# Attention cut into jobs of query tiles, with the first network's chunks at 256 and 320 tokens

## The chip, the cores and the metric
One core of a Trainium2 chip. The metric is the device time of one execution in microseconds; the kernel before takes 1015.93 us, the median of 3 runs (1014.83 to 1018.68).

## What is computed
Causal attention with a bias on 32 heads (batch 4 x 8 heads, 576 tokens, 64 wide), then two networks on the 2304 tokens of 512 values. All in float32.

```python
scores = scale * np.matmul(q, k.transpose(0, 1, 3, 2))
cum = np.cumsum(np.maximum(s, 0.0), axis=-1)
bias = -(cum[:, :, :, None] - cum[:, :, None, :])
scores = np.where(causal, -1000000000.0, scores + np.minimum(bias, 0.0))
attn = softmax(scores)          # exp(scores - max) / (sum + 1e-9)
x = np.matmul(attn, v)          # rearranged to (2304, 512)
h = np.maximum(np.maximum(x @ w1, x @ w2), x @ w3);  x = h @ w_out      # 512 -> 768 -> 512
y = ((x @ w_a) * (x @ w_b)) @ w_out2                                    # 512 -> 1536 -> 512
```

## The kernel before
Every float32 operand of a matmul is split into two parts that TensorE takes as float32r (hi and lo), so that a product is three matmuls (hi x hi, hi x lo, lo x hi) or, in attention, two with both parts stacked on the 128 rows of the contraction.

**Attention, a head at a time.** A head's 576 queries are 5 tiles of 128, 128, 128, 128 and 64 rows (`ROWS`), tile i against its `KEYS[i]` keys. VectorE splits q and k (`k_hi_copy` L720, `q_hi` L725, `split_k` L741, `split_q` L735). ScalarE writes the bias of each tile (`bias` L531, a Relu of the cumulative row, spread over 128 partitions by a DMA through `cum_dram`, with the tile's own value as bias), GpSimd puts the mask on the diagonal block (`mask` L470). TensorE makes the scores (L942, two matmuls a tile, four for the last), VectorE adds score and bias and reduces the extreme (`neg_scores` L755), ScalarE takes the exponential (L538), VectorE the reciprocal of the sums (L749), GpSimd multiplies (`normalise` L477), TensorE transposes 128x128 blocks, or 64-row ones in the last tile (L957), ScalarE and VectorE copy and split the transposes (`pt_hi` L548, L550; `pt_lo` L762, L766), TensorE multiplies with v (`output` L970), ScalarE and VectorE add the halves into `x_raw` (L558, L774). GpSimd also splits v (L489, L492).

**Slots.** All engines walk the same list of slots (`walk`). In slot n head n is scored and head n-1 is transposed and multiplied with v; head n+1's operands are prepared. Slots 0 to 8 hold attention alone. From slot 9 on four slots carry one chunk of 288 tokens of the first network: three with two of the 6 row blocks each (`up_part` L989, six parts of 12 matmuls a slot) and one with `down_part` (L1011, 72 matmuls). Attention's steps stand between the parts, and a part stands behind the last transposes, ahead of the output. Heads end at slot 32, so chunks 6 and 7 (slots 33 to 40) run alone. The order on each engine is written out by hand in its `slot` function; waits on semaphores are in the order of the instructions.

**Weights of the first network** come in 16 pieces of 768 columns: DMA into one of two buffers (`load_w1` L398), VectorE's copy `w1_hi` (L729), GpSimd's `w1_lo` (L483). Pieces 0 to 9 are split in slots 1 to 8, the rest in slots 9 to 11.

**Second network.** 6 chunks of 384 tokens (`CH2`), 12 row blocks each: 24 matmuls into `ab_ps` (L1073), then 12 into `out_ps` (L1084). The first network's result goes through DRAM (`y_dram`).

The output of a head, as it stands in the code:

```python
lo, hi = (0, SPLIT) if half == 0 else (SPLIT, SEQ)
todo = [(j, pt) for j in range(QT) if P * j < hi for pt in (pt_hi, pt_lo)]
for at, (j, pt) in enumerate(todo):
    q0 = max(lo, P * j)
    ins = nc.tensor.matmul(pv_ps[:, q0:hi], v_st[par][0:ROWS[j], j, :], ...)
```

## Time and profile before

| | |
|---|---|
| median of 3 runs | 1015.93 us |
| the profiled execution | 1014.57 us, span of its instructions 1012.6 us |
| TensorE busy | 972.7 us (96%), 6213 matmuls |
| VectorE, ScalarE, GpSimd busy | 481.4, 429.9, 237.1 us |
| granted clock of TensorE, mean | 0.976 of 2.4 GHz |
| moved by DMA | 64.11 MB |

Durations of instructions are those of one execution. A matmul's duration in the trace reaches over the start of the next, since they are pipelined; what one costs in a row of them is the distance of starts. "Busy" counts overlapping instructions once.

### The profile page before, as it was taken

What the parts mean: (1) busy time and instruction counts of PE and PEld (TensorE: products, weight loads), DVE (VectorE), ACT (ScalarE), POOL (GpSimd) and SP (SyncE); (2) the same over time, 40 slices, a digit from 0 to 9 for tenths busy, and PEclk for the clock granted to TensorE, in tenths of its full rate; (3) what the DMA queues carried; (4) which work ended last, traced back from release to release, by engine and by line L of the source; (5) the groups of instructions that cost most, each with busy time, mean ns of one, the idle gap of its engine ahead of it and who ended that gap; (6) DMA issues with size and microseconds to landing.
All of it is one profiled execution on the core that took longest, in us unless ns stands there. A gap on an engine that the chain in (4) does not pass through costs nothing.

```text
span 1012.6 us, 18390 instructions
## 1 busy us (share of the span) xinstructions
PE 972.7 (96%) x6213; PEld 942.9 (93%) x6213; DVE 481.4 (48%) x1151; ACT 429.9 (42%) x1070; POOL 237.1 (23%) x438
## 2 busy tenths in 40 slices
PE   3778799999999999999999999999999999999998
PEld 2666799999999999999999999999999999999998
DVE  6888788667667767664324543212112112112111
ACT  4677566666666666664133432112112112112111
POOL 4877864443443442441000000000000000000000
PEclk9976799999999999999999999999999999999999
DMA  7444542332332332300021431100100100100000
GB/s 190 115 128 131 139 123 67 90 78 74 80 83 69 82 96 52 102 8 24 1 102 60 153 125 47 62 0 0 62 0 8 54 0 16 46 0 26 5 0 31
DMA packets 31465, 64.11 MB, mean 63 GB/s; under 512 B 3712, under 2 KB 18048, under 8 KB 31424
## 3 DMA queue, kind: packets, MB, share of 16 engines
q1 hardware_dynamic: 31424, 63.60, 22.0%
q8 instruction: 21, 0.34, 0.1%
q14 instruction: 20, 0.16, 0.1%
HBM read 54.08 MB, written 9.51 MB: 63 GB/s over the span
## 4 chain that ended last, share of the span: by engine, by line
PE 88%; issue 0%; DVE 0%
PE bank L1073 30%; PE bank L989 23%; PE bank L1084 15%; PE bank L1011 8%; PE bank L970 5%; PE bank L942 5%; PE bank L957 4%; DVE soft L755 0%; DVE x_raw L774 0%; DVE o_stage L898 0%; DVE pt_lo L762 0%; DVE neg_max L755 0%
## 5 line engine op out<-in xcount | busy, mean ns | idle before, releaser
L888 DVE TENSOR_TENSOR g_raw<-bank,a_sb 128x384 f32<-128x384 f32 x72 | 40.2, 558 | 285.4 <-PE bank L1073 285.3
L989 PE MATMUL bank<-xs_hi,w_hi 128*128 128x288 f32 x576 | 174.1, 302 | 0.5 <-issue 0.5
L989 PE MATMUL bank<-xs_lo,w_hi 128*128 128x288 f32 x576 | 169.8, 295 | 0.0
L989 PE MATMUL bank<-xs_hi,w_lo 128*128 128x288 f32 x576 | 169.6, 294 | 0.0
L1073 PE MATMUL bank<-y_hi,w2b_lo 128*128 128x384 f32 x432 | 145.2, 336 | 0.0
L1073 PE MATMUL bank<-y_lo,w2b_hi 128*128 128x384 f32 x432 | 145.0, 336 | 0.0
L1073 PE MATMUL bank<-y_hi,w2b_hi 128*128 128x384 f32 x432 | 145.0, 336 | 0.0
L755 DVE CUSTOM_DVE_ANT_0 soft<-bank,soft 128x128 f32<-128x128 f32 (+4 forms) x160 | 86.4, 540 | 77.1 <-PE bank L942 53.5
L477 POOL TENSOR_SCALAR soft<-soft,rden 128x128 f32<-128x128 f32 (+4 forms) x160 | 99.0, 631 | 84.2 <-DVE rden L749 84.2
L538 ACT ACTIVATE soft<-soft,neg_max 128x128 f32<-128x128 f32 (+4 forms) x160 | 95.6, 598 | 43.6 <-DVE neg_max L755 43.4
L665 ACT ACTIVATE a_sb<-bank 128x384 f32<-128x384 f32 x72 | 35.3, 490 | 182.5 <-PE bank L1073 180.5
L989 PEld LDWEIGHTS bank<-xs_hi,w_hi 128*128 128x128 f32 x576 | 108.1, 188 | 3.5 <-issue 0.8
L989 PEld LDWEIGHTS bank<-xs_lo,w_hi 128*128 128x128 f32 x576 | 108.3, 188 | 0.8
L989 PEld LDWEIGHTS bank<-xs_hi,w_lo 128*128 128x128 f32 x576 | 108.2, 188 | 0.0
L669 ACT ACTIVATE g_hi<-g_raw 128x384 fp32r<-128x384 f32 x72 | 37.8, 525 | 163.8 <-DVE g_raw L888 163.8
L942 PE MATMUL bank<-k_hi,q_st 128*128 128x128 f32 (+2 forms) x192 | 75.7, 407 | 22.6 <-DVE neg_max L755 19.1
L531 ACT ACTIVATE soft<-cum_bc,cum_q 128x128 f32<-128x128 f32 (+4 forms) x160 | 90.0, 596 | 5.8 <-DMA cum_bc<-cum_dram 5.8
L548 ACT ACTIVATE pt_hi<-bank 128x256 fp32r<-128x256 f32 (+3 forms) x160 | 67.0, 420 | 56.1 <-PE bank L957 54.9
L470 POOL TENSOR_SCALAR_AFFINE_SELECT soft<-soft 128x128 f32<-128x128 f32 (+1 forms) x160 | 55.0, 355 | 138.9 <-ACT soft L531 130.8
L762 DVE TENSOR_TENSOR pt_lo<-bank,pt_hi 128x256 fp32r<-128x256 f32 (+3 forms) x160 | 73.0, 472 | 29.4 <-ACT pt_hi L548 24.2
L1073 PEld LDWEIGHTS bank<-y_hi,w2b_lo 128*128 128x128 f32 x432 | 81.2, 188 | 0.0
L1073 PEld LDWEIGHTS bank<-y_hi,w2b_hi 128*128 128x128 f32 x432 | 81.2, 188 | 0.0
(88 smaller groups left out, 2115.9 us busy)
## 6 DMA issues: line engine op xcount, KB each, us to landing
qk_raw<-in_qkT SPq DMA_DIRECT2D x64, 288.0 KB, 4.4
w_raw<-in_w SPq DMA_DIRECT2D x40, 384.0 KB, 3.4
cum_bc<-cum_dram SPq DMA_DIRECT2D x32, 288.0 KB, 3.4
v_raw<-in_v SPq DMA_DIRECT2D x32, 160.0 KB, 2.2
y_raw<-y_dram SPq DMA_DIRECT2D x6, 768.0 KB, 4.8
outT<-o_stage SPq DMA_DIRECT2D x24, 192.0 KB, 1.9
y_dram<-m_tmp SPq DMA_DIRECT2D x16, 144.0 KB, 1.8
y_dram<-h_raw SPq DMA_DIRECT2D x16, 144.0 KB, 1.8
```

Source lines behind the costliest of these rows:

```text
L470: nc.gpsimd.affine_select(out=diag, in_=diag, compare_op=ALU.is_ge, fill=masked, base=0, pattern=[[-1, r]], channel_multiplier=1).then_inc ...
L477: nc.gpsimd.tensor_scalar(part, part, rden[par][0:ROWS[i], i:i + 1], 1.0, ALU.mult, ALU.mult).then_inc(prob_done, 1)
L531: nc.scalar.activation(soft[par][0:ROWS[i], OFF[i]:OFF[i] + KEYS[i]], cum_bc[par][0:ROWS[i], 0:KEYS[i]], ACT.Relu, bias=cum_q[par][0:ROWS[ ...
L538: nc.scalar.activation(part, part, ACT.Exp, bias=neg_max[par][0:ROWS[i], i:i + 1], scale=-1.0, accum_out=sums[par][0:ROWS[i], i:i + 1]).th ...
L548: last = nc.scalar.activation(dst, src, ACT.Copy)
L755: nc.vector.tensor_tensor_reduce(part, score_ps[0:ROWS[i], at:at + KEYS[i]], part, 1.0, 3.0e38, ALU.add, ALU.min, neg_max[par][0:ROWS[i], ...
L762: last = nc.vector.tensor_tensor(pt_view(pt_lo, i, full), tr[:, 0:full * r].rearrange("p (j n) -> p j n", j=full), pt_view(pt_hi, i, full) ...
L942: ins = nc.tensor.matmul(score_ps[0:r, at + k0:at + k1], q_st[par][:, P * i:P * i + r], k[:, k0:k1], start=(part == 0), stop=(part == 1))
L989: ins = nc.tensor.matmul(up_ps[g], up1_w(w, f, g, kc), x[:, kc, :], start=(kc == 0 and at == 0), stop=(kc == KC - 1 and at == 2))
L1011: ins = nc.tensor.matmul(up_ps[j % 3], down1_w(w, f, j), h[:, f, :], start=(f == 0 and at == 0), stop=(f == FB1 - 1 and at == 2))
L1073: ins = nc.tensor.matmul(ab_ps[2 * (f % 2) + g], w2_cols(hi, f, (g * KC + kc) * P), y[:, kc, :], start=(kc == 0 and at == 0), stop=(kc == ...
L1084: ins = nc.tensor.matmul(out_ps[j], w2_cols(hi, f, 2 * KC * P + j * P), g[f % 2][:, :], start=(f == 0 and at == 0), stop=(f == FB2 - 1 and ...
```

## The change
- **Jobs.** Attention is 40 jobs instead of 32 heads: jobs 0 to 7 are heads 0 to 7 (batch 0) with query tiles 0 and 1 only (256 tokens), jobs 8 to 15 the same heads with tiles 2, 3 and 4, jobs 16 to 39 whole heads. Slots 0 to 8 are attention alone (`alone_slot`).
- **First network.** 8 chunks of 256 and 320 tokens in turn instead of 288. Chunk 0 starts at slot 9 and takes 8 slots, chunk 1 (slot 17) too: one row block a slot in six of them, half of the down part in two (`DENSE`). From slot 25 four slots a chunk, as before. Chunks 6 and 7 (slots 41 to 48) run alone.
- **Steps.** A slot has 6 steps; where it holds only three parts they stand at steps 0, 2 and 4, ahead of the transposes of that step. The output follows step 5. The weight pieces are split in slots 2, 4 (one each) and 8 to 14 (two each).
- **Bias as contraction rows.** `qk_st` has four planes: q_hi over q_lo, k_hi over k_hi; then the rows of the bias (cumulative sum and ones, hi and lo, 4 of the 64 upper rows, the others zero) over q_hi, and the same over k_lo. The scores hold the bias; `bias` and `mask` are gone, `neg_scores` adds a constant mask tile `causal` and scales by -SCALE. The four bias rows of all heads are made by VectorE at the start, go to DRAM and come back by two small DMAs a job (`load_bias`). GpSimd copies the upper halves (`upper`), ScalarE the lower (`lower`), VectorE subtracts twice (`split_q`, `split_k`).
- **Full shapes.** The last query tile is loaded as 128 queries from 448 on, of which the lower 64 partitions count (`TOP`, `QUERY`); its transposes and the last rows of v are 128x128 too.
- **Second network.** 5 chunks, four of 512 tokens and one of 256. Loops are unrolled, register waits are constants.

```diff
+N_JOBS = HEADS + N_HEADS
+EARLY_TILES, LATE_TILES = (0, 1), (2, 3, 4)
+    if n < HEADS:
+        return EARLY_TILES
+    return LATE_TILES if n < 2 * HEADS else tuple(range(QT))
-CH1 = SEQ // 2
+CHUNK = [((0, SPLIT), (SPLIT, SEQ))[c % 2] for c in range(N_CH1)]
+FIRST = [9, 17, 25, 29, 33, 37, 41, 45]
+DENSE = 2
-CH2 = 384
+CH2 = 512
+W1_PIECES = {2: [0], 4: [1], 8: [2, 3], 9: [4, 5], 10: [6, 7], 11: [8, 9], 12: [10, 11], 13: [12, 13], 14: [14, 15]}
...
             # scores
-                for k0, k1 in ((0, SPLIT), (SPLIT, SEQ)) if i == QT - 1 else ((0, KEYS[i]),):
-                    for part, k in enumerate((k_hi[par], k_lo[par])):
-                        ins = nc.tensor.matmul(score_ps[0:r, at + k0:at + k1], q_st[par][:, P * i:P * i + r], k[:, k0:k1],
+                    for part in range(2):
+                        ins = nc.tensor.matmul(score_ps[:, at + k0:at + k1], st[:, 2 * part, q0:q0 + P],
+                                               st[:, 2 * part + 1, k0:k1], start=(part == 0), stop=(part == 1))
...
             # transposes
-                    ins = nc.tensor.transpose(tr[0:w, j * r:(j + 1) * r], soft[par][0:r, at:at + w], ident[0:r, 0:r])
+                for j in reversed(range(i + 1)):
+                    ins = nc.tensor.transpose(tr[:, j * ROWS[i]:j * ROWS[i] + P], soft[m % 2][:, at:at + P], ident[:, :])
...
             # output: all 128 rows of v_st and pt
+                        ins = nc.tensor.matmul(pv_ps[:, q0:hi], v_st[m % 2][:, j, :],
+                                               pt[:, PT_STEP * j + q0:PT_STEP * j + hi],
...
             # reduction of the scores
+                nc.vector.tensor_tensor_reduce(scored(n, i), score_ps[TOP[i]:P, at:at + KEYS[i]],
+                                               causal[...], -SCALE, 3.0e38, ALU.add, ALU.min, ...)
...
             # start, VectorE
+            for b in range(2):
+                nc.vector.memset(qk_st[b][0:DH, 2:4, :].bitcast(F32), 0.0)
...
+            for b in range(2):
+                nc.vector.memset(qk_st[b][0:4, 2:4, :].bitcast(F32), 1.0).then_inc(st_init, 1)
...
             # TensorE, slots from 9 on
+                for step in range(STEPS):
+                    at = step if parts == STEPS else step // 2
+                    if parts == STEPS or step % 2 == 0:
+                        if rows:
+                            ups(n, at)
+                        else:
+                            down_part(c, downs[at])
+                    if live(m) and step in tr_step(m):
+                        transposes(m, tr_step(m).index(step))
+                    if live(n) and step in score_step(n):
+                        scores(n, 2 + score_step(n).index(step))
+                if live(m):
+                    output(m)
+                if live(n + 1):
+                    scores(n + 1, 0)
+                    scores(n + 1, 1)
```

## Rows read from the trace of the kernel before

**Rows 1.** Stages: length, busy us (instructions) of PE PEld DVE ACT POOL, clock, DMA
```profile
0.00:11.80 11.80, 1.91 (x9) 1.48 (x9) 6.61 (x20) 2.53 (x5) 1.42 (x10) 1.00 0.53 141
11.80:119.00 107.20, 80.81 (x343) 64.72 (x344) 87.07 (x216) 73.57 (x197) 82.76 (x131) 0.78 0.54 145
...
240.60:480.50 239.90, 239.90 (x1792) 232.00 (x1790) 158.59 (x434) 151.36 (x411) 89.96 (x189) 1.00 0.25 68
480.50:558.30 77.80, 77.25 (x579) 77.05 (x579) 25.97 (x52) 21.82 (x47) 0.00 (x0) 1.00 0.17 55
558.30:1012.60 454.30, 451.25 (x2592) 450.18 (x2591) 113.95 (x198) 100.77 (x195) 0.00 (x0) 1.00 0.11 35
```

**Rows 2.** The chain that ended last: its shares, then pieces (start, us, what)
```profile
PE 88%; issue 0%; DVE 0%
...
268.18 1.87 PE bank L970 x14
...
283.34 1.87 PE bank L970 x14
...
480.52 29.00 PE bank L989 x216
...
581.20 4.16 PE bank L1073 x24
...
1005.34 4.23 PE bank L1084 x24
```

**Rows 3.** TensorE in order of time in one mixed slot (start, us, instruction)
```profile
268.13 0.28 PE L970 MATMUL bank<-pt_lo,v_st 128*128 128x256 f32 x1
268.25 0.22 PE L970 MATMUL bank<-pt_hi,v_st 128*128 128x128 f32 x1
...
269.44 0.28 PE L970 MATMUL bank<-pt_lo,v_st 128*128 128x192 f32 x1
269.64 0.29 PE L970 MATMUL bank<-pt_hi,v_st 64*128 64x64 f32 x1
...
269.98 0.33 PE L942 MATMUL bank<-k_hi,q_st 128*128 128x128 f32 x1
...
278.39 0.60 PE L957 MATMUL bank<-ident,soft 128*128 128x128 f32 x4
278.75 0.36 PE L942 MATMUL bank<-k_hi,q_st 128*64 128x256 f32 x1
...
281.04 0.51 PE L957 MATMUL bank<-ident,soft 64*128 64x64 f32 x5
281.49 0.40 PE L989 MATMUL bank<-xs_hi,w_hi 128*128 128x288 f32 x1
```

**Rows 4.** Groups by line: instruction, count, busy us, mean ns, idle before and releasers
```profile
L531 ACT ACTIVATE soft<-cum_bc,cum_q 128x128 f32<-128x128 f32 (+4 forms) x160 | 90.0, 596 | 5.8 <-DMA cum_bc<-cum_dram 5.8
L755 DVE CUSTOM_DVE_ANT_0 soft<-bank,soft 128x128 f32<-128x128 f32 (+4 forms) x160 | 86.4, 540 | 77.1 <-PE bank L942 53.5 <-issue 15.6 <-POOL soft L470 6.1
L762 DVE TENSOR_TENSOR pt_lo<-bank,pt_hi 128x256 fp32r<-128x256 f32 (+3 forms) x160 | 73.0, 472 | 29.4 <-ACT pt_hi L548 24.2 <-ACT pt_hi L550 4.1
L741 DVE TENSOR_TENSOR k_lo<-qk_raw,k_hi 128x576 fp32r<-128x576 f32 x32 | 26.2, 820 | 0.0
L483 POOL TENSOR_TENSOR w_lo<-w_raw,w_hi 128x768 fp32r<-128x768 f32 (+1 forms) x16 | 30.6, 1911 | 0.0
```

**Rows 5.** VectorE at the start, in order of time
```profile
0.94 0.54 DVE L701 MEMSET x_raw<- 32x576 f32 x1 [0.94 <-PEq L1126]
...
11.76 0.29 DVE L755 CUSTOM_DVE_ANT_0 soft<-bank,soft 128x128 f32<-128x128 f32 x1 [1.75 <-POOL soft L470]
```

**Rows 6.** TensorE in a slot of attention alone: last transposes, then the output
```profile
98.44 0.49 PE L957 MATMUL bank<-ident,soft 64*128 64x64 f32 x5 [0.36 <-DVE pt_lo L762]
...
100.13 0.36 PE L970 MATMUL bank<-pt_hi,v_st 128*128 128x256 f32 x1 [0.55 <-issue]
```

**Rows 7.** DMA issues: line, engine, count, KB each, us to landing
```profile
w_raw<-in_w SPq DMA_DIRECT2D x40, 384.0 KB, 3.4
```

More of the change, by code:

```diff
@@ L590, in slot @@
                 if live(m - 1):
-                    other_half(m - 1, par == 0)
+                    other_half(m - 1)
+                if ahead_of(n) is not None:
+                    for kc in range(KC - 1):
+                        x_hi(ahead_of(n), kc)
+                if live(m):
+                    for k in range(len(tiles(m))):
+                        pt_hi_copy(m, k)
+                exp(n, 2)
+            def slot(n):
+                m = n - 1
+                c, e = place(n)
+                rows, downs, rest, ahead, early = rows_of(n), downs_of(n), rest_of(n), ahead_of(n), early_w2(n)
+                if live(m - 1):
+                    other_half(m - 1)
@@ L626, in slot @@
[L626 to L632 removed]
+                    if rows and i == 0 and rest is None:
+                        m_copy(c, rows[0])
+                    if len(rows) == 2 and i == 3:
+                        m_copy(c, rows[1])
@@ L840, in slot @@
+            def slot(n):
+                m = n - 1
+                c, e = place(n)
+                rows, downs, rest, ahead, early = rows_of(n), downs_of(n), rest_of(n), ahead_of(n), early_w2(n)
+                for piece in W1_PIECES.get(n, []):
+                    w1_hi_copy(piece)
+                neg_scores(n, 0)
+                if live(m - 1):
+                    x_add(m - 1)
                 if rest is not None:
                     x_lo(rest, KC - 1)
-                if before(up, down) is not None:
-                    h_lo_sub(*before(up, down))
+                if pending_row(n) is not None:
+                    h_lo_sub(*pending_row(n))
```

1052 lines of the change are left out of this document (509 added, 543 removed).

## The prediction, made before the changed kernel was run
> **What bounds the kernel now.** I read the table of stages first, then the chain of waits, then single slots of TensorE. The table [rows 1] cuts the 1012.6 us span into five parts: 11.8 us of start; 107.2 us in which attention runs with no matmul of the first network beside it (TensorE at a mean granted clock of 0.78, VectorE busy 87.07 us of it); slots that mix attention and the first network up to 480.5 us (four of its six chunks are in the third row: PE busy 239.90 of 239.9 us at clock 1.00); 77.8 us of chunks 6 and 7 of that network alone; 454.3 us of the second network. The chain [rows 2] is 88% TensorE. So from 119 us on TensorE is the bound and only fewer or cheaper matmuls help; before that it is a pipeline of five engines in which VectorE works 81% of the time, and there TensorE's time is partly thrown away. That is the place where time can be won: work of the first network put beside attention earlier.
>
> **TensorE's prices.** Chunk 6 does 216 matmuls of 288 columns in 29.00 us (134 ns each), the second network 24 of 384 columns in 4.16 us (173.3 ns) [rows 2]. The difference of 39 to 40 ns is 96 columns at 2.4 columns per ns, so one costs columns/2.4 plus a fixed 13.3 ns. That gives 120.0 ns for 256 columns, 146.7 for 320, 226.7 for 512. The 256-column matmul from 268.13 to 268.25 us agrees [rows 3].
> A full attention head in a mixed slot costs TensorE 283.34 - 268.18 = 15.16 us, less 72 x 0.1333 = 9.60: 5.56 us [rows 2].
>
> **Second network.** 6 chunks x 432 matmuls of 384 columns become 4 x 432 of 512 and 432 of 256. Before: 2592 x 0.1733 = 449.3 us. After: 1728 x 0.2267 + 432 x 0.120 = 391.7 + 51.8 = 443.5. **-5.8 us**, from 432 fewer fixed parts. What lies around (454.3 - 449.3 = 5.0 us, three of them the tail) stays. Bounds: if the fixed part grew with the columns (173.3/384 per column, 231.1 ns at 512) the gain would be 0, with none at 512 columns it would be 5.8 + 1728 x 0.0133 = 29; two widths on one line make me take -5.8. The wider evictions (up to four 512-column copies per chunk and engine) lie beside 8.2 us of matmuls per block: nothing.
>
> **First network alone.** Chunks of 256 and 320 columns keep the sum of columns and the number of matmuls: 288 x (0.120 + 0.1467) = 76.8 us against 77.8 with its waits. 0.
>
> **Full shapes.** The last query tile is 64 rows, and its matmuls use part of the array. The 64-row transposes: from 281.04 to 281.49 us, with 0.09 us lost in front (the last full matmul would end at 280.95) and 0.1 us behind; four full ones from 278.39 to 278.75, so five full ones are about 0.45 too; what goes is some 0.1 us [rows 3]. The two 64-row matmuls of the output: 269.44 + 0.10 to 269.98 is 0.44 us; two full-height ones, bounded by weight loads of about 0.11, take 0.22, and the first scores matmul behind them loses its 0.04. Together **-0.36 us** per full head, in 16 heads that lie in purely TensorE-bound slots (-5.8 us) and in the mixed slots below. 5.56 becomes 5.2. Bounds 0 to -0.6.
> The Trainium skill, "TensorE: Matmul & The Clock Gate", section "Back-to-back issue gap", speaks against this part: it lists up to 64 columns at about 60 cycles and 128 columns at 134, so five transposes widened from 64 to 128 columns would cost 5 x 31 ns = 0.15 us more by an estimate from that page, and 0.36 would shrink to 0.2. The rows show 0.09 us for a 64-wide and 0.09 for a 128-wide transpose [rows 3], so I go by the rows.
>
> **Bias as contraction rows.** It removes per head five Relu passes of ScalarE (90.0 us / 32 = 2.8 us), GpSimd's five masks and one copy, and the wait of mask and scores on them; VectorE's four passes of 576 columns (L741's takes 0.82 us) become two of the same width: at most -1.6 us, and as two of the four are plain copies and cheaper I take -1.1 [rows 4]. ScalarE and GpSimd each get a copy of up to 1152 columns (1.3 to 1.8 us). None of it is on TensorE's path in the old mixed slots, where all three had slack, so there it is worth 0; its worth is that slots may be shorter. Scores keep their number of matmuls.
>
> **Start.** VectorE gets four memsets of 1152 columns before the scan (one of 576 took 0.54 us [rows 5], so 1.0 each), four passes for the bias rows (2.4 us), then a larger store to DRAM and a reload. The old first score reduction starts at 11.76 us [rows 5] behind a similar bounce; mine at 15. **+3.3** (0 to +6, by how much of it hides behind loads).
>
> **Attention alone.** Before 107.2/9 = 11.9 us a slot. After: 8 slots with tiles 0 and 1 only, one (slot 8) with three tiles, two weight pieces and three splits of x. A two-tile slot: VectorE has at most 2/5 of L755 and L762 (0.9 + 0.7), two splits of 256 columns (0.9), x (0.4), reciprocal (0.35): 3.3 us, at 81% busy 4.1; two fifths of 11.9 is 4.8 [rows 1, 4]. The chain (transposes, two copies, output, scores, reduction, exp) doesn't shrink with the tile, so I take 4.6: 8 x 4.6 = 37, less 2 for the first; slot 8 costs 3/5 of 11.9 and 1: 8. The first network then starts at 15 + 35 + 8 = **58 us, where it was 119**.
>
> **The 16 new dense slots (9 to 24)**, chunks 0 and 1 at half density, 36 matmuls a slot.
> Slots 9 to 16: 36 x 0.120 = 4.3 us, three tiles 3.9 us (5.2 less two score tiles, two transposes and the first output half). The last transposes now stand directly ahead of the output with no matmuls between. In the old slots with nothing between but four scores, TensorE went from 98.44 (transposes) to 100.13 (output) [rows 6]: some 1.3 us idle if the scores are not there. 9.5 us. Six of these slots carry two weight pieces: GpSimd 2 x 1.9 us, and each buffer waits for 3.4 us of DMA before VectorE's copy, the first thing in its slot [rows 4, 7]. GpSimd sums to about 9.1 us. I take 10.3 there: 6 x 10.3 + 2 x 9.6 = 81.
> Slots 17 to 24: 36 x 0.1467 = 5.3, attention 5.2, the idle 1.3, waits of scores on reductions 0.2: 12.0 each, 96. VectorE needs some 8 us of 12.
> Chunk 2 thus starts at 58 + 81 + 96 = 235 us.
>
> **The rest of the mixed slots**: chunks 2 to 5, 16 slots: 72 matmuls each, 8 x 8.64 + 8 x 10.56 = 153.6, and 16 x 5.2 - 1.5 (the last has no scores) = 81.7. End at 470 us, where it was 480.5.
>
> **Sum** on the span: 470 + 77.8 + (454.3 - 5.8) = 996.5, against 1012.6: **-16**. The profiled execution took 1014.57 us (2 us around its span), so it would be 998.5; the median of the runs shown is 1015.93, some 1.4 above it, and I forecast **1000 us**. Most of the gain is not a gain in full: the 61 us earlier start are paid back by 177 us of dense slots that hold a quarter of the first network.
>
> **Rivals.**
> (a) *The dense slots run slowly because the clock falls.* They leave 1 to 2 us idle per slot, and in the old attention-only stage, where TensorE waits in every slot, the granted clock was 0.78 on the mean; with the two levels 2.4 and 1.2 GHz that is 1.2 GHz in 44% of the time [rows 1]. If half of the 8 to 10.5 us of TensorE work in each of the 16 slots ran at 1.2 GHz, each gets 4.7 us longer: +75, about 1075. It decides against the change at +16/16 = 1.0 us per slot, i.e. about one slot in five at the low clock throughout. Against it: here TensorE works 85% at full clock, there about half. The Trainium skill, "TensorE: Matmul & The Clock Gate" (section "HAM oscillation — how this bites in real kernels"), has waits between bursts of matmuls throwing the clock back; rows 1 agree for the stage before. Chance 0.13, most likely at 1018 to 1045.
> (b) *Muted:* shapes and widths bring nothing (+11.6), or weight pieces set slots 9 to 14 at 11.9: 1008 to 1016, say 1011. That full shapes don't remove the gaps, since the gap after each transpose group is of another kind, belongs here. Chance 0.17.
> (c) *Better:* two-tile slots at 4.1 (-4), no idle ahead of the output (-10 or so over 16 slots since the scores' waits overlap it), 985. For it: all helpers got lighter. Chance 0.18.
> (d) The forecast, 990 to 1008: 0.52.
>
> Range: 984 to 1022, which leaves out the rest of (a) and a little of (c). Half a percent (5 us) is about what can be told from no change. Faster takes (c), (d) and a third of (b): 0.76; same, the rest of (b), 0.11; slower 0.13.
>
> **What would show it.** Right: first matmul of the first network near 58 us; slots 17 to 24 near 12 us with one idle of 1.3 us ahead of the output's matmuls; granted clock 1.00 from there on; no 64-row matmul; 24 matmuls of 512 columns in 5.44 us; chunk 6 at 470. Wrong: clock under 0.9 between 60 and 235 us, waits of VectorE on the weight DMA in each slot from 9 to 14, a first reduction later than 18 us, or 512-column matmuls of 231 ns.

## The result, and the profile after

The changed kernel takes **1028.01 us** (median of 4 runs, 1027.53 to 1028.70) beside 1016.44 us for the kernel before on the same chip: ratio **1.0113 [1.0092, 1.0134]**. It is 1.1% slower, where the forecast was 1000 us in a range of 984 to 1022.

TensorE has less to do than before and the kernel is longer all the same: 5776 matmuls instead of 6213, busy 949.7 us instead of 972.7. The page of the kernel after, its first section and its chain:

```profile
PE 949.7 (93%) x5776; PEld 864.0 (84%) x5776; DVE 475.4 (46%) x1059; ACT 393.9 (38%) x896; POOL 221.6 (22%) x306
PE 87%; issue 5%; DVE 3%; DMA 1%; ACT 1%; POOL 1%; SPq 0%; ACTq 0%; POOLq 0%; DVEq 0%
```

Before, from 113 us on (its 88% of the span), the chain was almost TensorE's alone [rows 2]. The chain after is followed to the start, and 11% of the span on it are other engines and "issue". To see where, the stages of the kernel after (columns as in [rows 1]: length, busy us and count of PE, PEld, DVE, ACT, POOL, granted clock, DMA):

```profile
16.50:66.80 50.30, 27.31 (x96) 21.25 (x97) 36.57 (x107) 25.10 (x73) 29.04 (x46) 1.00 0.46 142
66.80:160.50 93.70, 75.53 (x533) 71.94 (x532) 68.31 (x147) 49.59 (x112) 62.26 (x62) 0.95 0.34 106
160.50:266.30 105.80, 89.83 (x619) 83.69 (x617) 72.06 (x183) 63.62 (x157) 43.83 (x66) 1.00 0.21 66
266.30:501.20 234.90, 234.86 (x1795) 233.04 (x1794) 153.82 (x392) 135.29 (x340) 79.86 (x121) 1.00 0.18 54
...
579.00:1026.30 447.30, 443.81 (x2161) 376.19 (x2159) 107.80 (x164) 95.11 (x165) 0.00 (x0) 1.00 0.11 36
```

These are: attention alone, slots 9 to 16, slots 17 to 24, the four-slot chunks and the second network; the first network alone, left out here, is 77.8 us. From the fourth row on TensorE is hardly ever idle (3.5 us in the second network). In the second and third row it idles 18 and 16 us.

The same work in the kernel before has to be cut elsewhere. When its slot 17 starts, heads 0 to 15 and chunks 0 and 1 are done; after, that is the state at 266.3 us:

```profile
0.00:240.30 240.30, 204.02 (x1254) 183.36 (x1255) 182.64 (x466) 155.75 (x417) 146.87 (x249) 0.90 0.43 115
240.30:480.50 240.20, 240.20 (x1794) 232.30 (x1792) 158.82 (x436) 151.54 (x412) 90.26 (x190) 1.00 0.25 68
```

| like for like | before | after | |
|---|---|---|---|
| heads 0 to 15, chunks 0 and 1 | 240.3 | 266.3 | **+26.0** |
| heads 16 to 31, chunks 2 to 5 | 240.2 | 234.9 | -5.3 |
| first network alone | 77.8 | 77.8 | 0 |
| second network | 454.3 | 447.3 | -7.0 |
| span | 1012.6 | 1026.3 | +13.7 |

Behind 266.3 us the change won about what was forecast. The first quarter lost 26 us, though TensorE was busy for less time in it (193.87 us of the first 266.30 after, 204.02 of the first 240.30 before) and its granted clock was higher (0.98 beside 0.90).

### The profile page after: what moved, and what is told of

Its sections match the earlier page's. It is cut to its first block, busy times and chain, and to the rows that moved or that the text cites. A ratio compares the mean times of both kernels' runs of the same rounds, so it can differ in the third digit from the quotient of the medians.

```text
span 1026.3 us, 15198 instructions
## 1 busy us (share of the span) xinstructions
PE 949.7 (93%) x5776; PEld 864.0 (84%) x5776; DVE 475.4 (46%) x1059; ACT 393.9 (38%) x896; POOL 221.6 (22%) x306
## 4 chain that ended last, share of the span: by engine, by line
PE 87%; issue 5%; DVE 3%; DMA 1%; ACT 1%; POOL 1%; SPq 0%; ACTq 0%; POOLq 0%; DVEq 0%
PE bank L1047 29%; PE bank L946 21%; PE bank L1062 14%; PE bank L965 7%; PE bank L898 6%; PE bank L928 6%; PE bank L914 4%; DVE soft L723 1%; DMA w_raw<-in_w 1%; DVE qk_st L690 1%; ACT qk_st L495 1%; POOL w_lo L460 0%; POOL soft L454 0%; DVE qk_st L696 0%; DVE pt_lo L732 0%
## 5 line engine op out<-in xcount | busy, mean ns | idle before, releaser
L946 PE MATMUL bank<-xs_hi,w_hi 128*128 128x256 f32 (+1 forms) x576 | 174.3, 303 | 0.7 <-ACT h_raw L543 0.7
L946 PE MATMUL bank<-xs_hi,w_lo 128*128 128x256 f32 (+1 forms) x576 | 171.3, 297 | 0.0
L946 PE MATMUL bank<-xs_lo,w_hi 128*128 128x256 f32 (+1 forms) x576 | 171.3, 297 | 0.0
L454 POOL TENSOR_SCALAR soft<-soft,rden 128x576 f32<-128x576 f32 (+4 forms) x160 | 93.0, 599 | 257.2 <-DVE rden L709 257.2
L898 PE MATMUL bank<-qk_st 128*128 128x256 f32 (+4 forms) x384 | 97.8, 367 | 45.6 <-DVE neg_max L723 16.5
L1047 PE MATMUL bank<-y_lo,w2b_hi 128*128 128x512 f32 (+1 forms) x360 | 132.5, 368 | 0.0
L1047 PE MATMUL bank<-y_hi,w2b_hi 128*128 128x512 f32 (+1 forms) x360 | 132.5, 368 | 0.0
L1047 PE MATMUL bank<-y_hi,w2b_lo 128*128 128x512 f32 (+1 forms) x360 | 132.5, 368 | 0.0
L504 ACT ACTIVATE soft<-soft,neg_max 64x576 f32<-64x576 f32 (+4 forms) x160 | 96.1, 601 | 78.3 <-DVE neg_max L723 77.2
L723 DVE CUSTOM_DVE_ANT_0 soft<-bank,causal 64x576 f32<-64x576 f32 (+4 forms) x160 | 86.5, 540 | 59.9 <-PE bank L898 58.5
L928 PE MATMUL bank<-pt_hi,v_st 128*128 128x320 f32 (+4 forms) x224 | 61.3, 297 | 26.9 <-issue 24.8
```

The source lines that it names most:

```text
L454: nc.gpsimd.tensor_scalar(part, part, rden[n % 2][:, i:i + 1], 1.0, ALU.mult, ALU.mult).then_inc(prob_done, 1)
L504: nc.scalar.activation(scored(n, i), scored(n, i), ACT.Exp, bias=neg_max[n % 2][TOP[i]:P, i:i + 1], scale=-1.0, accum_out=sums[n % 2][TOP[ ...
L723: nc.vector.tensor_tensor_reduce(scored(n, i), score_ps[TOP[i]:P, at:at + KEYS[i]], causal[TOP[i]:P, ZERO + P - KEYS[i]:] if i < QT - 1 el ...
L898: ins = nc.tensor.matmul(score_ps[:, at + k0:at + k1], st[:, 2 * part, q0:q0 + P], st[:, 2 * part + 1, k0:k1], start=(part == 0), stop=(pa ...
L928: ins = nc.tensor.matmul(pv_ps[:, q0:hi], v_st[m % 2][:, j, :], pt[:, PT_STEP * j + q0:PT_STEP * j + hi], start=(at == 0), stop=(at == len ...
L946: ins = nc.tensor.matmul(up_ps[g][:, 0:width1(c)], up1_w(w, f, g, kc), x[:, kc, 0:width1(c)], start=(kc == 0 and at == 0), stop=(kc == KC ...
```

## Where the first quarter went: two readings

**A loop that goes once around in each dense slot.** The chain of waits through one of slots 17 to 24 in the kernel after, from one output (L928) to the next:

```profile
197.99 1.94 PE bank L928 x14
...
200.47 1.76 PE bank L946 x12
...
203.81 0.19 ACT soft L504
...
205.46 0.75 DVE qk_st L690
206.24 0.42 DVE pt_lo L732
...
207.32 0.80 PE bank L898 x4
208.12 1.76 PE bank L946 x12
209.88 0.55 PE bank L914 x5
210.43 1.10 issue
211.52 1.94 PE bank L928 x14
...
214.05 1.15 ACT qk_st L495
215.22 0.48 ACT h_hi L538
```

211.52 less 197.99 is 13.53 us, the length of slots 18 to 22 (the first and the last two of the eight are shorter, the mean is 13.1 to 13.2). Two of the slot's three groups of 12 first-network matmuls lie on this chain, one on that of the next slot; between them it passes through VectorE, ScalarE and "issue". In the next slot it leaves TensorE right behind the output and four scores, for ScalarE's L495. What releases ScalarE stands in its own rows, again in order of time, with the idle time and its releaser in brackets:

```profile
199.97 0.65 ACT L518 ACTIVATE pv_tmp<-bank 64x576 f32<-64x576 f32 x1 [1.72 <-PE bank L928]
200.64 1.17 ACT L495 ACTIVATE qk_st<-qk_raw 64x1152 fp32r<-64x1152 f32 x1
```

The head of ScalarE's queue in a slot is `other_half`, the copy of the output just made. It waits for the last matmul of the output, and the copy of the next job's operands (`lower`, L495), the split of the first network's row block and the exponentials stand behind it. VectorE's h_lo and second reduction wait for that, then the exponentials, the transposes' copies, the last scores, the last transposes and the output again. TensorE is busy 11.29 us of such a slot, the loop lasts 13.5. With 72 first-network matmuls a slot (chunks 2 to 5) TensorE's own work is longer than the loop, and it doesn't show.

**GpSimd's subtraction holds VectorE.** Two equal passes of VectorE on 64x256, then what GpSimd did, in a slot with one weight piece:

```profile
36.19 0.42 DVE L690 TENSOR_TENSOR qk_st<-qk_raw,qk_st 64x256 fp32r<-64x256 f32 x1
36.53 2.02 DVE L696 TENSOR_TENSOR qk_st<-qk_raw,qk_st 64x256 fp32r<-64x256 f32 x1
```
```profile
36.23 2.04 POOL L460 TENSOR_TENSOR w_lo<-w_raw,w_hi 128x768 fp32r<-128x768 f32 x1 [0.68 <-DVE w_hi L701]
```

The second pass lasts until 0.28 us after the end of GpSimd's. In slots 9 to 14 there are two pieces. Slot 10 is the longest of them (13.3 us, the others 11.6). Its subtraction of the next job's q (L690) stands ahead of the third reduction (L723) and is held; in slot 11, with the same list, L690 starts 0.45 us earlier in its slot, between GpSimd's two passes, and gets through in 0.57 us, and the k pass (L696) is held, behind that reduction. VectorE's rows of slot 10, then of slot 11:

```profile
84.18 1.81 DVE L690 TENSOR_TENSOR qk_st<-qk_raw,qk_st 64x320 fp32r<-64x320 f32 x1
86.02 0.76 DVE L723 CUSTOM_DVE_ANT_0 soft<-bank,causal 64x576 f32<-64x576 f32 x1
...
97.06 0.57 DVE L690 TENSOR_TENSOR qk_st<-qk_raw,qk_st 64x320 fp32r<-64x320 f32 x1
...
98.36 1.60 DVE L696 TENSOR_TENSOR qk_st<-qk_raw,qk_st 64x576 fp32r<-64x576 f32 x1
```

GpSimd's pass for slot 10 runs from 82.01 to 85.64, and the held one ends 0.35 us after it. The delayed reduction delays its exponential, behind which ScalarE's `pt_hi` copies are queued, and so the output: TensorE idles 3.24 us ahead of it in slot 10 and 1.57 in slot 11.

```profile
82.01 3.63 POOL L460 TENSOR_TENSOR w_lo<-w_raw,w_hi 128x768 fp32r<-128x768 f32 x2
```
```profile
89.86 0.38 PE L928 MATMUL bank<-pt_hi,v_st 128*128 128x320 f32 x1 [3.24 <-issue]
```

L690 is late where TensorE's clock falls early in the slot. Stages of one slot each (from one reciprocal of VectorE to the next): slots 10, 11 and 12 of the kernel after, then slot 11 of the run with 384 columns below, whose code is the same up to the second network:

```profile
76.53:89.87 13.34, 10.10 (x67) 9.69 (x67) 9.13 (x19) 5.98 (x13) 8.73 (x8) 0.87 0.49 148
89.87:101.52 11.65, 10.08 (x67) 9.68 (x67) 8.89 (x19) 5.86 (x13) 9.10 (x8) 0.85 0.34 101
101.52:113.10 11.58, 8.80 (x67) 8.26 (x67) 9.23 (x20) 5.99 (x13) 9.02 (x8) 1.00 0.42 129
88.92:102.48 13.56, 10.35 (x67) 9.81 (x67) 9.28 (x20) 5.75 (x13) 8.94 (x8) 0.87 0.48 148
```

In slots 9 to 14 of the kernel after the granted clock falls to 1.2 GHz for a stretch three times, at 77.1, 90.7 and 114.6 us, each time soon after TensorE had been idle for 1.9 to 3.2 us ahead of an output. Where the stretch begins within 0.6 us of the slot's start the scores come late, L690 meets GpSimd's second pass, and the slot takes 13.3 to 13.6 us; where it begins later (slots 11 and 13) the slot stays at 11.6. At clock 1.00 none of slots 9 to 14 was longer than 11.7 in either run. In the profile with 384 columns four slots, 11 to 14, are long, and the six together last 77.1 us instead of 71.3, with the same code: a single profile is no sure measure of these slots.

These gave the first theories. T1: the weight pieces' subtraction on GpSimd makes the early slots long. T2: slots 17 to 24 are a loop through the output. The rival to both was that VectorE or ScalarE simply have too much in these slots, and for the second network that its gain comes from something other than the width.

## The experiments

All are edits of the kernel after, except where the kernel before is named. Times are medians, ratios are to the kernel before on the same chip; the kernel after is at 1028.01 and 1.0113. The kernel before had medians of 1014.51 to 1016.65 us on the chips of these runs, so differences of medians between kernels of different chips are sure to about 2 us only, and the ratios are to be preferred. Line numbers shift by a few with an edit. "Slots 17 to 24" is read from the distance of VectorE's reciprocals (0.19 us each, one a slot).

### 384 columns in the second network
```diff
-CH2 = 512
+CH2 = 384
```


> The changed kernel with the second network's chunks set back to 384 tokens (six chunks instead of five), all else as changed. By the sum of the prediction the 432 matmuls more cost 13.3 ns each: +5.8 us against the changed kernel, about 1034 us. Rival: the wider evictions or the larger loads had taken the gain away, then 0 (about 1028).

1035.92 us, 1.0194 [1.0164, 1.0223]. TensorE's blocks of 24 matmuls are 4.16 us in this kernel and 5.44 in the kernel after (chain of waits).

The second network takes 452.3 us (585.86 to 1038.2) instead of 447.3: the width is worth **5.0 us**. The other 2.0 of the 7.0 come with the rest of the change to that part (unrolled loops, constant waits); they were not tested apart. The rest of the 7.9 us between the medians lies ahead of 579 us, which this edit doesn't touch. In the profiled execution (1040.28 us, the longest of the four) that part is 6.9 us longer: slots 11 to 14 take 13.4 to 13.6 us at clock 0.87, as told above.

### Low parts of the weights by VectorE, right behind its copy
```diff
             def w1_hi_copy(piece):
...
+                dve.wait_ge(w1_hi_done, piece + 1)
+                nc.vector.tensor_tensor(w1_lo[:, cols], w1_raw[piece % 2][:, :], w1_hi[:, cols].bitcast(F32),
+                                        ALU.subtract).then_inc(w1_lo_done, 1)
...
-                for piece in W1_PIECES.get(n, []):
-                    w1_lo_sub(piece)
```


> The changed kernel with the low parts of the first network's weights subtracted by VectorE right behind its copy, instead of by GpSimd. Theory 1: GpSimd's 1.9 us subtraction holds VectorE's subtractions up (2.03 us instead of 0.42 for a split in the slots with a piece), and that sets the slots with pieces: slots 2 and 4 get 1.5 us shorter each, slot 8 by 2, slots 9 to 14 by about 1 each, in all -9 to -13 us (about 1017), although VectorE gets 16 x 0.95 = 15 us more work. Rival: VectorE's own load or the weight DMA sets these slots, then 0 to +8 us.

1038.67 us, 1.0228 [1.0196, 1.0259]: worse. Slots 2 and 4 with one piece are 0.5 us or so shorter, but slots 9 to 14 take 12.5 to 15.5 us instead of 11.6 (12.5 and 13.0 in slots 9 and 10, at clock 1.00; 13.6 to 15.5 in the four others, at 0.78 to 0.88). Slots 17 to 24 are untouched at 13.55. So the place matters: two copies and two subtractions at the head of VectorE's queue stand in the loop. This doesn't refute the hold; it shows that the repair can't stand there.

### ScalarE's `lower` behind the first copy of the transposes
```diff
-                if live(n + 1):
-                    lower(n + 1)
...
                         pt_hi_copy(m, tr_step(m).index(i))
+                    if live(n + 1) and i == 0:
+                        lower(n + 1)
```
(VectorE's two splits stand one step later.)

> The changed kernel with ScalarE's copy of the lower halves (1.15 us) moved from the head of its slot to behind the first copy of transposes, and VectorE's two splits one step later each; only in slots from 9 on. Theory 2: in slots 17 to 24 the chain copy, h_hi, h_lo, second reduction, exp, m_copy, pt_hi, pt_lo, split, fourth reduction, last scores leaves TensorE idle 2 us a slot in the middle; with the copy and a split out of it these 8 slots fall from 13.5 to 11.6 to 12.2 us: -10 to -15 us in all (about 1015). Rival: other work in the same queues takes their place, under -4 us.

1026.81 us, 1.0100 [1.0069, 1.0131]; slots 17 to 24 alternate between 12.5 and 13.6 us. It takes 1.15 us off the queue's head and brings about one.

### A part of the matmuls behind the last transposes
```diff
-                    at = step if parts == STEPS else step // 2
-                    if parts == STEPS or step % 2 == 0:
+                    at = step if parts == STEPS else {0: 0, 2: 1, 5: 2}.get(step)
+                    if at is not None:
```


> The changed kernel with the third part of 12 matmuls in slots 9 to 24 moved from ahead of the last transposes to behind them. Theory 3: nothing covers the two copies between the last transposes and the output (TensorE idle 1.1 to 3.2 us there in each slot); with 1.4 or 1.8 us of matmuls in between, 16 slots get 1.1 to 1.4 us shorter, -18 us (about 1010). Rival: these slots are set by VectorE's and ScalarE's order, so TensorE's wait only moves to the scores or transposes: under -5 us.

1024.71 us, 1.0095 [1.0062, 1.0128]; slots 18 to 22 are 13.03 us instead of 13.53. The gap of 1.1 us ahead of the output is filled, and half a microsecond comes of it.

### Both


> The changed kernel with both edits of the two runs before: the copy and splits later, and the third part of matmuls behind the last transposes. Alone they brought 1 and 3 us. Theory 2+3 (each wait stands in the other's shadow): slots 17 to 24 have 5.3 us of chunk, 5.2 of attention and some 1 us left, 11.6 to 12 each instead of 13.5, and slots 9 to 16 lose 0.5 each: -14 to -18 us, about 1012. Rival: the effects add and no more, -4 to -5 us, then what sets these slots is neither.

1028.12 us, 1.0122 [1.0096, 1.0148]; slots 18 to 22 are 13.3 us. Together they bring nothing. ScalarE's head of the queue still stands waiting for the output, now for 3.38 us where it was 1.72. In this profile the clock also fell to 0.89 in slot 25, which took 15.8 us instead of 14.2; that is more than the 1.1 us that slots 17 to 24 won together.

```profile
201.53 0.65 ACT L518 ACTIVATE pv_tmp<-bank 64x576 f32<-64x576 f32 x1 [3.38 <-PE bank L928]
```

### No low parts at all
GpSimd writes zeros in place of the low parts of the first network's weights, so that part of the computation is left out.
```diff
-                nc.gpsimd.tensor_tensor(w1_lo[:, cols], w1_raw[piece % 2][:, :], w1_hi[:, cols].bitcast(F32),
-                                        ALU.subtract).then_inc(w1_lo_done, 1)
+                nc.gpsimd.memset(w1_lo[:, cols].bitcast(F32), 0.0).then_inc(w1_lo_done, 1)
```


> The changed kernel where GpSimd writes zeros for the low parts of the first network's weights instead of subtracting (this leaves out the low parts of these weights): one write-only pass in place of one that reads two operands from SBUF. Theory 1: the subtraction holds VectorE's passes up. The splits in slots 2 and 4 fall from 2.03 us to 0.42 to 1, slots 2, 4 and 8 get 1.5 us shorter each, and slots 9 to 14 by 0.5 to 1.5: -8 to -13 us. Rival, that VectorE's order alone or the DMA of the pieces sets them: under -3 us.

1020.87 us, 1.0054 [1.0035, 1.0073]: 7.1 us less. Slots 2 and 4 take 6.1 and 4.85 us (7.7 and 6.6 after), slot 8 takes 9.7 (12.1). Slot 10 falls from 13.3 to 11.6, and no slot from 8 to 14 has a clock under 1.00. But the others of slots 9 to 14 stay at 11.6 (slot 9 at 11.2). Their chain has no weight piece in it; it is the loop of slots 17 to 24 with fewer parts:

```profile
83.81 1.15 ACT qk_st L494
...
87.11 0.80 PE bank L897 x4
...
91.76 1.77 issue
```

T1 holds for slots 2, 4, 8 and 10 and fails, on this evidence, for the rest of slots 9 to 14.

### Full height of the output in the kernel before
```diff
+            for pt in (pt_hi, pt_lo):
+                nc.vector.memset(pt[DH:P, (PT_STEP + P) * (QT - 1):].bitcast(F32), 0.0)
...
-                    ins = nc.tensor.matmul(pv_ps[:, q0:hi], v_st[par][0:ROWS[j], j, :],
-                                           pt[0:ROWS[j], PT_STEP * j + q0:PT_STEP * j + hi],
+                    ins = nc.tensor.matmul(pv_ps[:, q0:hi], v_st[par][:, j, :],
+                                           pt[:, PT_STEP * j + q0:PT_STEP * j + hi],
```


> The kernel before with one part of the change alone: the last two matmuls of each head's output at the full height of 128 rows, over zeros, instead of 64. By the sum of the prediction 0.22 to 0.26 us less in each of the 23 heads that lie in slots bound by TensorE, and less than that in the 9 alone: -5 to -6 us, ratio 0.994 to 0.995. Rival: the lost time belongs to the wait of the weight loads and stays: 0.

1006.29 us (1005.26 to 1008.34), 0.9909 [0.9884, 0.9935]: **8.2 us from one matmul call of the kernel before**, and two memsets at the start that put zeros into the rows it now reads. The same stretch as in [rows 3], TensorE in order of time:

```profile
267.44 0.27 PE L972 MATMUL bank<-pt_lo,v_st 128*128 128x192 f32 x1
267.56 0.22 PE L972 MATMUL bank<-pt_hi,v_st 128*128 128x64 f32 x1
...
267.72 0.30 PE L944 MATMUL bank<-k_hi,q_st 128*128 128x128 f32 x1
```

From the 192-column matmul to the scores 0.28 us, where it was 0.54 [rows 3]: 0.26 us a head. In 24 heads beside the first network that is 6.2 us, and chunk 6 starts 6.2 us earlier (474.34 us, before 480.52 [rows 2]). Next to nothing lies behind that: the two profiled executions differ by the same 6.2 us (1008.34 and 1014.57), and the other 2.0 are the scatter of the runs, the profiled one of 1008.34 being the longest of its four.

### Full density from slot 13 and 21 on, attention alone between
```diff
-FIRST = [9, 17, 25, 29, 33, 37, 41, 45]
-DENSE = 2
+FIRST = [13, 21, 25, 29, 33, 37, 41, 45]
+DENSE = 0
...
-    return list(range(STEPS // 2 * (e - FB1), STEPS // 2 * (e - FB1 + 1))) if c < DENSE else list(range(STEPS))
+    return list(range(STEPS)) if e == 3 else []
```


> The changed kernel with the jobs as they are but chunks 0 and 1 at full density: chunk 0 in slots 13 to 16 and chunk 1 in slots 21 to 24, two row blocks a slot, and slots 9 to 12 and 17 to 20 attention alone. Theory 4: a slot has a floor of some 10 us from its chain whatever it holds, and the 16 half-dense slots (199.5 us) sit on it with TensorE idle; packed, slots 9 to 12 take 9 to 10 us, 13 to 16 12.5, 17 to 20 10 to 11, 21 to 24 15.8, in all 189 to 197: -3 to -10 us. Rival: attention alone runs at a falling clock and is slower than half-dense slots, +5 to +20 us.

1045.08 us, 1.0296 [1.0270, 1.0322]. Slots 17 to 20 hold no matmul of the first network, and still take 9.8, 13.4, 11.9 and 13.9 us. A loop is there with nothing of the first network on it:

```profile
176.73 3.50 PE bank L928 x14
...
186.10 1.33 PE bank L898 x4
187.43 1.07 PE bank L914 x5
```

Output to output is 12.86 us (176.73 to 189.59). This doesn't stand alone as a measure of the loop: the granted clock is 0.81 in that stretch (156 to 209 us), and output, scores and transposes take 5.90 us here and 3.29 in the chain of the kernel after, so that at full clock the loop would be some 10.3, an estimate from these rows. It shows that a slot has a floor: the 5.3 us of first-network matmuls in slots 18 to 22 of the kernel after add some 3.2 to it and not 5.3. The rival named ahead of the run came true, too: the clock was 0.63, 0.50 and 0.75 in slots 10 to 12, which hold attention alone, and slots 9 to 24 took 217 us instead of 199.

### The next job's first scores ahead of the output
```diff
-                if live(m):
-                    output(m)
                 if live(n + 1):
                     scores(n + 1, 0)
                     scores(n + 1, 1)
+                if live(m):
+                    output(m)
```


> The changed kernel with the next job's first two scores moved from behind the output to ahead of it, in all slots from 9 on; only TensorE's order. Theory 5: a slot's length is a loop, from one output through the next job's scores, VectorE's and ScalarE's queues, to the next output, 11.6 us plus the output's 1.94, whatever the slot holds of the first network. Taking the output out of the first part of the loop and filling TensorE's idle ahead of it makes slots 17 to 24 1 to 2 us shorter each and slots 9 to 16 0.5 to 1.5: -12 to -25 us, about 1010. Rival: the head of ScalarE's queue (its copy of the output's half) still waits for the output, so the loop stays: 0 to -5 us.

1029.05 us, 1.0107 [1.0087, 1.0128]; slots 18 to 22 are still 13.53 to 13.57 us. The first reduction could start earlier now, but ScalarE's head of the queue keeps the loop shut; its pieces of the chain:

```profile
200.38 0.02 ACT pv_tmp L518
...
201.05 1.16 ACT qk_st L495
```

### That, and the heads of the queues cleared
`other_half` (ScalarE) and `x_add` (VectorE) of the last output stand behind the second exponential and the second reduction.
```diff
-                if live(m - 1):
-                    other_half(m - 1)
...
                 if rest is None:
                     exp(n, 1)
+                    if live(m - 1):
+                        other_half(m - 1)
...
-                if live(m - 1):
-                    x_add(m - 1)
...
+                if rest is None and live(m - 1):
+                    x_add(m - 1)
```


> As the run with the scores ahead of the output, and besides ScalarE's copy of the output's half and VectorE's addition of it moved from the head of their slots to behind the second exp and the second reduction (except in the first slot of a chunk that needs the head at once). Theory 5: now nothing at the heads of the queues waits for the output, the loop loses its 1.94 us and 1.15 us of copy: slots 17 to 24 at 11 to 11.8 (5.3 + 5.2 of TensorE work are the floor), slots 9 to 16 at 9.5 to 10.5: -28 to -38 us, about 995. Rival: VectorE's order alone sets them: -5 us or less.

1019.33 us (10 runs), 1.0029 [1.0017, 1.0040]; slots 18 to 22 12.44 us, chunk 6 at 492.00 us instead of 501.20. Beside the kernel above, which did nothing, 9.7 us.

### And a part behind the last transposes


> The run before with the third part of 12 matmuls behind the last transposes too (slots 9 to 24). By theory 5, with the loop out of the way, what is left idle ahead of the output (0.5 to 1 us) is covered: 0 to -8 us more. Rival: no effect or some us slower, as the reductions of the first network's rows come later in VectorE's queue.

1010.73 us, **0.9930 [0.9912, 0.9947]**, the first version of the change that beats the kernel before. Slots 18 to 22 take 11.40 us and are TensorE's from end to end, with 0.2 us idle (chain, output to output; what is left out are TensorE's pieces and 0.04 of issue). All eight slots take 90.4 us instead of 105.2.

```profile
202.55 1.94 PE bank L932 x14
204.49 1.84 PE bank L950 x12
...
213.76 0.19 issue
213.95 1.95 PE bank L932 x14
```

This settles T2: three moves, of which two did next to nothing alone (+1.0 and -3.3 us, ratios that overlap with that of the kernel after) and the third was not run alone, take 17.3 us together, and no work was taken from any engine, which rules out the rival of too much work for slots 17 to 24. Slots 9 to 14 are still 11.7 us, and now the weight pieces are on their chain (VectorE's two subtractions of q and k, 1.94 and 1.49 us on the chain; they take 0.49 and 0.75 us where GpSimd writes zeros):

```profile
82.92 1.94 DVE qk_st L692
...
85.66 1.49 DVE qk_st L698
```

### The kernel before with full height and 512 columns
```diff
-CH2 = 384
+CH2 = 512
```
(with the edit of full height above, loops unrolled where their width changes)

> The kernel before with two parts of the change alone: the output at full height, and the second network in four chunks of 512 tokens and one of 256. The output alone brought 8 us, and the wider chunks 7 to 8 in the changed kernel: about 1000 us, ratio 0.985. Rival: the wider chunks brought their gain only together with the rest, then 0.991.

1005.56 us (1004.33 to 1007.01), 0.9877 [0.9858, 0.9897]. Beside full height alone the width brings 0.7 us in the medians, 3 by the ratios; the second network takes 451.6 us (553.48 to 1005.1) instead of 454.3, 2.7 less. Its blocks of 24 matmuls of 512 columns last 5.51 us here and 5.44 in the kernel after, 2.9 ns a matmul; why was not found out. Over 1728 such matmuls that is 5.0 us, so the same width is worth less here. Two small parts of the change, on the kernel before, give 1005.56, the whole change 1028.01.

### The best order without low parts
The edits of the 1010.73 us version, and zeros for the low parts of the first network's weights, which leaves that part out of the computation.

> The run with the heads reordered and the third part behind the transposes, and GpSimd writing zeros for the low parts of the first network's weights (it leaves these low parts out). Theory 1: with the loop gone, slots 9 to 14 stay at 11.7 us because GpSimd's subtraction holds VectorE's splits (1.94 us in the chain instead of 0.5); without it they fall to 9.8 to 10.7, slots 2 and 4 by 2 to 3 us, slot 8 by 3: -12 to -17 us, about 996. Rival: slots 9 to 14 stay at 11.7 as in the changed kernel without the subtraction (11.6 there), then -7 as there.

996.82 us, 0.9815 [0.9799, 0.9832], 13.9 us less than with them (11.7 by the ratios), where the same edit was worth 7.1 (6.0) on the kernel after. Slots 9 to 14 fall to 10.3 us (two of them to 10.6 and 10.9). So T1 was right for them too, and the earlier failure was the loop's shadow: with the loop alone the slots took 11.6 us, with the hold alone 11.7, and taking one away left the other. At 10.3 us the chain that leads to 91.8 us goes through GpSimd's queue and then a load into one of the two weight buffers:

```profile
87.22 4.53 DMA w_raw<-in_w
```

### The best order with the weights split otherwise, nothing left out
High parts by ScalarE (one at the head of its slot, one after the first group, or at steps 0 and 2), low parts by VectorE in the middle of its slot; GpSimd has none.
```diff
-                for piece in W1_PIECES.get(n, []):
-                    w1_hi_copy(piece)
...
+            def w1_low(n, at):
+                for piece in W1_PIECES.get(n, [])[at:at + 1]:
...
+                    if i in (1, 3):
+                        w1_low(n, i // 2)
...
+            def w1_high(n, at):
+                for piece in W1_PIECES.get(n, [])[at:at + 1]:
...
+                    if i in (0, 2):
+                        w1_high(n, i // 2)
```


> The run with the heads reordered and the third part behind the transposes, with ScalarE making the high parts of the first network's weights and VectorE the low parts in the middle of its slot; nothing left out, GpSimd has no weights. Theory 1: the hold on VectorE goes (1.5 us a slot) for 0.6 us more of its own work and with 1.3 us less at its head: slots 9 to 14 at 10.5 to 11.2, slots 2 and 4 1.5 us shorter: -5 to -10 us, about 1003. Rival: VectorE's sum sets slots 9 to 14: +3 to +12 us, as when it had both passes (13.7 us a slot).

**999.58 us** (999.22 to 999.90), **0.9840 [0.9824, 0.9857]**: faster than both kernels, with the whole computation. Slots 9 to 14 take 10.7 to 11.5 us (the longest two at clock 0.85), slots 18 to 22 11.40, chunk 6 starts at 473.48 us. Where VectorE's low parts at the head of its queue cost 10.7 us over the kernel after, the same passes spread through the slot, with the copies taken off it, save 11.2 over the version that leaves them on GpSimd. What is left in slots 9 to 14 is one idle ahead of the output:

```profile
79.24 2.15 issue
```

How much of this is owed to the jobs and the bias rows? Chunk 6 starts here at the first of these rows, and in the kernel before with full height and 512 columns at the second (at 474.34 us with full height alone):

```profile
473.48 26.05 PE bank L954 x216
475.86 28.88 PE bank L996 x216
```

That is 0.9 to 2.4 us for all that the change does ahead of chunk 6, about what medians of the kernel before differ by from chip to chip. The spans of the two are 998.1 and 1005.1 us, and 4.8 of these 7.0 us lie in the second network (446.8 and 451.6 us), which neither jobs nor bias rows touch.

## Why the prediction was wrong, step by step

**Right.** The prices of TensorE: blocks of 216 matmuls take 26.05 us at 256 columns and 31.92 at 320, 120.6 and 147.8 ns (forecast 120.0 and 146.7), and 24 of 512 columns 5.44 us, 226.7 ns, as forecast. Chunks 2 to 5 took 234.9 us (235.3): less 153.6 for the first network at the forecast price that leaves 81.3 for 16 heads less 1.5, so 5.2 us a head, where it was 5.56. The first network alone 77.8 (77.8). The second 447.3 (448.5): mis-sized by little, 5.0 from the width, where 5.8 stood, and 2.0 from unrolling, where nothing stood. Full shapes: 0.26 us of a head came from the output's two matmuls and the scores behind them, as in the working (0.22 and 0.04), and the kernel before gains 6.2 us of its profile by that alone. The transposes were not run apart, but the chains show them: before, the five 64-row ones take 0.45 us and the 12 matmuls behind them 1.78 where such groups take 1.59; after, the five full ones take 0.55 and the group behind them is no longer than the others. That is the 0.1 us of the working.

**Wrong.** All of the miss lies ahead of 266.3 us, 31.3 us in three terms; less the 1.6 us won over the forecast behind that point it is the 29.8 us between the forecast span (996.5) and the real one, to a rounding of the sum.

1. *"The first network starts at 58 us": 66.8, 8.8 late.* The start was about right: the first reduction came at 15.8 (15 forecast). Two-tile slots without a weight piece took 4.3 us (4.6 forecast). The failing part is that a two-tile slot was costed without its weight piece, and slot 8 at three fifths of an old one plus 1: slots 2 and 4 took 7.7 and 6.6 us, slot 8 took 12.1 instead of 8. Without GpSimd's subtraction they were 6.1, 4.85 and 9.7.
2. *"Slots 9 to 16: 6 x 10.3 + 2 x 9.6 = 81": 93.7, 12.7 over.* The working had GpSimd's 9.1 us and the DMA's 3.4 as the possible bounds, looked at each engine's sum, and not at what GpSimd does to VectorE nor at the loop. Each of these two alone gives 11.6 to 11.7 us. With both away the slots take 10.3: the forecast, reached with zeros in place of the low parts. Of the 12.7 us 1.7 are slot 10's, in which the hold met a fallen clock.
3. *"5.3 + 5.2 + the idle 1.3 + waits 0.2: 12.0 each": 13.53 in slots 18 to 22, 9.8 over in all eight.* This is the step that failed in kind. The sum took TensorE's work and added one idle, read from a slot of the old attention-only stage [rows 6]. The idle ahead of the output was 1.10 us, close to the forecast 1.3, and it was only one of several on a closed chain: TensorE was busy 11.29 us of a slot and idle 2.25, where the sum had 10.5 and 1.5. A slot that isn't bound by TensorE has to be costed as its loop: from the output through the first entries of ScalarE's and VectorE's queues to the next output. With that loop opened the slots took 11.40, under the forecast 12.0: 5.3 of the first network, 5.9 of attention and 0.2 idle. The 5.2 us for attention held in chunks 2 to 5 and not here: the output takes 1.94 us instead of 1.71, the scores 2.08 instead of 1.89, the transposes 1.82 instead of 1.65.

**The rivals.** The sign of rival (a) came true, its mechanism only in a small part: the granted clock was 0.95 in slots 9 to 16, where it helped to make slot 10 longer by 1.7 us, and 1.00 in slots 17 to 24, and these eight slots were 1.2 us over each all the same. Its break-even of 1.0 us a dense slot was right, and passed by another route: 22.5 us over in 16 slots. Rival (b) named weight pieces that set slots 9 to 14 at 11.9, which came close (11.6), but had no case with slots 17 to 24 affected too. No rival had a slower kernel by this mechanism, though the old attention-only slots of 11.9 us with TensorE busy 75% [rows 1] were the sign of it: there too a slot took what its loop takes. The change cuts 8 heads into 16 jobs, and a job pays for a slot.

**Where the expected gain went.** Started 52 us earlier (66.8 instead of 119), the first network's first two chunks lasted 16 slots instead of 8. A dense slot saves TensorE's idle time only if the rest of the slot is shorter than TensorE's share. In the kernel after it was longer in all 16. With the order of the queues mended and the weight split moved the kernel takes 999.58 us, beside 1005.56 for the kernel before with full height and wide chunks, 0.9840 [0.9824, 0.9857] and 0.9877 [0.9858, 0.9897]. The intervals just miss each other, and by the ratios the difference is 3.8 us, no more than the 4.8 by which the second networks of the two differ. So that jobs and bias rows pay is not shown: ahead of chunk 6 the largest part of the diff is worth 0.9 to 2.4 us, about the scatter.

**Open.** What makes up the 2.15 us left ahead of the output in slots 9 to 14 of the best version. Why a 512-column matmul costs 2.9 ns more in the kernel before with wide chunks. The two queue heads were not moved one without the other, so their shares aren't known. What the jobs and what the bias rows are worth by themselves, since neither was run alone.

## What to carry to other kernels

A slot of a software pipeline costs the longer of its bound engine's work and its closed loop, and the loop is found by following one result around until it comes back to itself, through whatever stands at the head of each in-order queue. Cutting the work into more and lighter slots buys that loop more often; before doing it, move whatever waits for the slot's last result away from the queue heads. When two limits are equally long, each edit alone shows nothing: undo them together before calling either innocent. And compare a large change stage by stage with the best small part of it: here one matmul call at full height brought the kernel before about as far, up to chunk 6, as all of the jobs and bias rows did.

## What the runs showed of the hardware

**A GpSimd subtraction holds a VectorE pass, and it depends on where the operands lie.** A VectorE subtraction of 64x256 with both inputs in SBUF took 0.42 us, and 2.02 us beside a GpSimd subtraction of 2.04 us; passes with an input in PSUM kept their time: the 64x576 reduction took 0.760 us on the mean in the first 160 us and 0.760 from 280 us on, where GpSimd does no such subtraction (0.76 also in slot 11, from 97.67 us, with GpSimd at its subtractions from 95.44 to 99.35), and the 128x384 `pt_lo` 0.558 and 0.551, while the 64x576 subtraction of k took 1.60 us in slots 11 to 14 and 0.76 late in the kernel. The Trainium skill, "SBUF — State Buffer", section "Who interferes with whom", says that a VectorE instruction with two SBUF inputs contends with a GpSimd instruction that reads SBUF, and not with one that only writes. Both halves agree with the rows: in slot 9 of the kernel with zeros VectorE's subtraction keeps its plain 0.49 us in the middle of GpSimd's writes.

```profile
64.66 1.42 POOL L460 MEMSET w_lo<- 128x768 f32 x2
65.09 0.49 DVE L689 TENSOR_TENSOR qk_st<-qk_raw,qk_st 64x320 fp32r<-64x320 f32 x1
```

**Two matmuls on 64 of 128 rows between full ones cost 0.26 us a head more than full-height ones** (0.54 us from the 192-column matmul to the scores behind them, 0.28 with full height), though the full ones work on twice the rows. The Trainium skill, "TensorEngine Tiling (Array Packing)", section "Key Properties", has a change of the tiling mode drain TensorE; it gives no time for it. That this is what was seen was not tested apart.

**A fixed part of 13.3 to 14.4 ns a matmul** over columns/2.4, at granted clock 1.00, held from 256 to 512 columns in the kernel after and its edit with 384 (120.6, 147.8, 173.3 and 226.7 ns at 256, 320, 384 and 512). The Trainium skill, "TensorE: Matmul & The Clock Gate", section "Back-to-back issue gap", gives about 2.5 ns for it, for the gap of a single matmul; these blocks measure five times that, and the measurement decides. In the kernel before with wide chunks it was 16.3 ns at 512 columns (229.6 ns). That it doesn't grow with the columns in the kernel after is what its wider chunks live on.
